# Attention outputs per head in two column halves of the TensorE array, written in one burst per unit

## The reference, cut to what matters

```python
def _attn_ref(q, k, v):                       # B, H, S, D = 4, 8, 576, 64
    q_d, k_d, v_d = (means over 4 neighbouring rows of q, k, v)      # 144 rows each
    out_d  = softmax(q_d @ k_d.T / 8) @ v_d                          # coarse, 144 keys
    mask   = np.abs(pos[:, None] - pos[None, :]) < 4
    out_local = softmax(where(mask, q @ k.T / 8, -1e9)) @ v          # a band of 7 keys
    return np.repeat(out_d, 4, axis=2) + out_local

def reference(...):
    x = attention output as (B*S, H*D) = (2304, 512)
    h = x @ w_in;  g = max(h, 0) + alpha * min(h, 0);  y = g @ w_out         # 512 -> 2048 -> 512
    h = y @ w2_in; u = h if h > 0 else exp(h) - 1;     return u @ w2_out     # 512 -> 2048 -> 512
```

## Time and profile before

| what | before |
|---|---|
| median of three runs | 945.79 us (945.70 to 945.86) |
| the profiled execution | 946.88 us, span 945.1 us |
| PE, PEld busy | 934.2, 882.3 us |
| DVE, ACT, POOL busy | 566.5, 328.8, 285.3 us |
| granted PE clock | 1.0 in every slice |

### The profile page before, as it was taken

How to read it: one execution, slowest core, us unless ns; L and a number is a source line. 1 busy time by engine, 2 the same in 40 slices (tenths; PEclk the granted TensorE clock), 3 DMA queues, 4 the chain that set the end, 5 groups by cost and what they waited for, 6 DMA issues and landing times.

```text
span 945.1 us, 15299 instructions
## 1 busy us (share of the span) xinstructions
PE 934.2 (99%) x5615; PEld 882.3 (93%) x5620; DVE 566.5 (60%) x1100; ACT 328.8 (35%) x756; POOL 285.3 (30%) x395
## 2 busy tenths in 40 slices
PE   8999999999999999999999999999999999999998
PEld 6999999999999999999999998888888888898887
DVE  5875666665565555445446566565856566756563
ACT  5853334333342313133232123232533233523233
POOL 3898952222112225455457552110001100000000
PEclk9999999999999999999999999999999999999999
DMA  7755522211211103536335234434454444454411
GB/s 168 166 146 142 144 72 53 52 41 40 50 41 39 28 16 112 156 107 195 101 134 201 60 119 112 122 112 119 116 180 122 112 122 113 153 149 112 122 45 68
DMA packets 119834, 100.70 MB, mean 107 GB/s; under 512 B 66000, under 2 KB 82384, under 8 KB 119760
## 3 DMA queue, kind: packets, MB, share of 16 engines
q1 hardware_dynamic: 118576, 99.42, 37.6%
q10 hardware_dynamic: 1184, 0.30, 0.2%
HBM read 80.29 MB, written 19.40 MB: 105 GB/s over the span
## 4 chain that ended last, share of the span: by engine, by line
PE 90%; POOL 5%; issue 2%; DVE 2%; ACT 1%; DMA 1%; SPq 0%; DVEq 0%; POOLq 0%; ACTq 0%
PE ps L236 27%; PE ps L237 26%; PE ps L238 26%; PE ps L469 3%; PE ps L436 2%; PE ps L461 1%; POOL w_out_lo L718 1%; POOL w_in_lo L718 1%; PE ps L418 1%; PE ps L426 1%; POOL p_l L692 1%; POOL vd L684 1%; PE ps L443 1%; PE ps L451 1%; POOL p_c L689 1%
## 5 line engine op out<-in xcount | busy, mean ns | idle before, releaser
L238 PE MATMUL ps<-common,w_hi 128*128 128x384 f32 x768 | 258.2, 336 | 0.0
L237 PE MATMUL ps<-common,w_hi 128*128 128x384 f32 x768 | 257.9, 336 | 0.0
L237 PEld LDWEIGHTS ps<-common,w_hi 128*128 128x128 f32 x768 | 144.7, 188 | 0.0
L238 PEld LDWEIGHTS ps<-common,w_hi 128*128 128x128 f32 x768 | 144.3, 188 | 0.0
L311 ACT ACTIVATE common<-act_g 128x384 fp32r<-128x384 f32 x96 | 50.4, 525 | 245.8 <-PE ps L238 125.5
L236 PE MATMUL ps<-common,w_out_lo 128*128 128x384 f32 x384 | 132.7, 346 | 0.4 <-DVE common L315 0.4
L236 PE MATMUL ps<-common,w_in_lo 128*128 128x384 f32 x384 | 132.6, 345 | 0.0
L869 ACT ACTIVATE act_g<-act_g 128x384 f32<-128x384 f32 x96 | 50.5, 526 | 196.0 <-DVE act_g L865 196.0
L236 PE MATMUL ps<-w_hi,common 128*128 128x512 f32 x288 | 113.8, 395 | 1.7 <-ACT xT L324 1.0
L238 PE MATMUL ps<-w_hi,common 128*128 128x512 f32 x288 | 113.5, 394 | 0.0
L237 PE MATMUL ps<-w_out_lo,common 128*128 128x512 f32 x288 | 113.5, 394 | 0.0
(11 more groups left out here) (103 smaller groups left out, 1615.2 us busy)
## 6 DMA issues: line engine op xcount, KB each, us to landing
ring<-w_in_parts SPq DMA_DIRECT2D x168, 256.0 KB, 2.7
w_in_parts<-parts SPq DMA_DIRECT2D x8, 1280.0 KB, 5.7
qk_nat<-in_q SPq DMA_DIRECT2D x32, 144.0 KB, 2.8
v_nat<-in_v SPq DMA_DIRECT2D x16, 288.0 KB
out<-xT SPq DMA_DIRECT2D x18, 256.0 KB, 2.2
qk_nat<-in_k SPq DMA_DIRECT2D x30, 144.0 KB, 3.3
v_blk<-in_v SPq DMA_DIRECT2D x64, 67.5 KB
xT<-in_moe_w_in SPq DMA_DIRECT2D x16, 256.0 KB, 3.0
```

The costliest lines, as they stand in the source:

```text
L237: pe.matmul(psum, l_hi, r_lo, start=False, stop=False)
L238: return pe.matmul(psum, l_hi, r_hi, start=False, stop=stop)
```

## The change

For each head the outputs are computed in one half of the array's columns: head 0 writes partitions 0 to 63 of the result and head 1 partitions 64 to 127, for the coarse and for the local part.

- `v_win` replaces `v_blk`: v as it is, 64 columns per head as stationary operand, windows padded from 54 to 64 partitions (`KP`). The zero blocks move to the probabilities: `pT_l` gets a side dimension, and the moving operand has 2 x 48 columns, of which each window sees its own. `vd` holds one copy.
- A matmul of the local outputs has 64 stationary and 96 moving columns (128 and 48 before), one of the coarse outputs 64 and 144 (128 and 144 before). Their numbers stay: 12 and 4 a unit. In the built program they stand on tiles of 128 x 64 of the array, at column 0 for head 0 and at column 64 for head 1, taking turns; all other matmuls stay on 128 x 128.
- `OUTPUTS` becomes two jobs, `O` 0 (coarse and the first block of 2 x 96 columns) and `O` 1 (the other two blocks), and `bursts` never splits them. The step has 13 jobs instead of 14, still seven bursts.
- DVE: `copy_coarse` is one operation of 128 x 144, `write_x` one of 128 x 192 for `O` 0 and two for `O` 1. In the mixed part `sum_local` and `reciprocals` of unit u + 1 stand ahead of `copy_coarse` at `O` 0.
- ACT: `copy_pT_local` has two operations of 64 partitions instead of one of 108. The high parts of the weights leave ACT.
- POOL: `sum_v` has three operations instead of four. `hi_of_weights` is on POOL for all chunks, in two operations of 512 columns (one of 1024 on POOL before).

```diff
-            v_blk = sb("v_blk", [2 * KW, NWH, HEADS, 2, D])
-            vd = sb("vd", [SC, HEADS, 2, 2, D])
+            v_win = sb("v_win", [2 * KP, NWH, HEADS, D])
+            vd = sb("vd", [SC, HEADS, 2, D])
...
-            pT_c, pT_l = sb("pT_c", [SC, 2, NW, HEADS, DQ]), sb("pT_l", [2 * KW, NWH, HEADS, QW])
+            pT_c, pT_l = sb("pT_c", [SC, 2, NW, HEADS, DQ]), sb("pT_l", [2 * KP, NWH, 2, HEADS, QW])
...
-                for h in range(HEADS):
-                    for x in range(2):
-                        last = pe.matmul(ps[:, bank, h * SD:(h + 1) * SD], vd[:, h, x, :, :].rearrange("p o d -> p (o d)"),
-                                         pT_c[:, x, :, h, :], start=x == 0, stop=x == 1)
-                last.then_inc(oc_done, 1)
-
-            def output_local(pe, u, h, bank):
-                pe.wait_ge(v_win_loaded, V_LOADS * (u + 1))
-                pe.wait_ge(ptl_copied, 2 * u + 2)
-                for i in range(NWH):
-                    last = pe.matmul(ps[:, bank, QW * i:QW * (i + 1)],
-                                     v_blk[:, i, h, :, :].rearrange("p s d -> p (s d)"), pT_l[:, i, h, :],
-                                     start=True, stop=True)
-                last.then_inc(ol_done, 1)
+                for x in range(2):
+                    for h in range(HEADS):
+                        pe.matmul(ps[D * h:D * (h + 1), bank, 0:SD], vd[:, h, x, :], pT_c[:, x, :, h, :], start=x == 0,
+                                  stop=x == 1)
+
+            def output_blocks(pe, u, n, bank):
...
+                for j in range(NBH):
+                    if block_at(j)[0] == n:
+                        for i in (2 * j, 2 * j + 1):
+                            for h in range(HEADS):
...
+                                last = pe.matmul(to, v_win[:, i, h, :], pT_l[:, i, :, h, :], start=True, stop=True)
+                last.then_inc(o_done, 1)
...
-                elif kind == "OC":
-                    copy_coarse(dve, u)
-                    if BATCH_UNITS <= u and u + 1 < UNITS:
-                        if u + 2 == UNITS:
-                            sum_local(dve, u + 1, 0)
-                        sum_local(dve, u + 1, 1)
-                        reciprocals(dve, u + 1)
-                elif kind == "OL":
+                elif kind == "O":
+                    if i == 0:
+                        if BATCH_UNITS <= u and u + 1 < UNITS:
+                            if u + 2 == UNITS:
+                                sum_local(dve, u + 1, 0)
+                            sum_local(dve, u + 1, 1)
+                            reciprocals(dve, u + 1)
+                        copy_coarse(dve, u)
                     write_x(dve, u, i)
...
-            def hi_of_weights(act, c):
-                act.wait_ge(w_loaded[c % WS], 32 * (c // WS + 1))
-                act.activation(w_hi[:, :, c, :], w_stage[:, c % WS, :, :], ACT.Copy).then_inc(w_hi_done, 1)
+            def hi_of_weights(gp, c):
+                gp.wait_ge(w_loaded[c % WS], 32 * (c // WS + 1))
+                for which in range(2):
+                    last = gp.tensor_scalar(w_hi[:, which, c, :], w_stage[:, c % WS, which, :], 1.0, 0.0, ALU.mult, ALU.add)
+                last.then_inc(w_hi_done, 1)
```

More of the change, by code:

```diff
@@ L171, in bursts @@
         grouped = [jobs[sum(sizes[:n]):sum(sizes[:n + 1])] for n in range(len(sizes))]
[L172 removed]
+        burst = []
+        for job in jobs[sum(sizes):]:
+            if len(burst) == 2 or burst and job[1:3] == OUTPUTS[0]:
+                grouped.append(burst)
+                burst = []
+            burst.append(job)
+        return grouped + [burst]
     with ExitStack() as ctx:
```

131 lines of the change are left out of this document (67 added, 64 removed).

## The result

| | before | after |
|---|---|---|
| median | 945.83 us (945.70 to 945.87, 4 runs) | 932.58 us (931.34 to 933.37, 4 runs) |
| profiled execution, span | 946.88, 945.1 us | 933.14, 931.3 us |

The ratio is 0.9859, with a 95% interval of 0.9842 to 0.9876. The forecast of 931.0 us is 1.6 us off and the range holds the time, but not every step behind it was right: two large ones were wrong in opposite directions. The kernel before ran 38 times beside this kernel and those of the experiments; seven of these executions took 948.9 to 950.2 us at a mean granted clock of 0.996 to 0.998, the others 945.4 to 946.5, and none of the seven was profiled.

The account below looks back on a forecast made before the run. PE, busy 934.2 of 945.1 us, was taken as the bound except in units 0 to 3 and at unit 5's wait. 946.88 - 16.8 (outputs) + 0.8 (POOL) + 1.2 (clock) = 932.1; median 1.1 lower, 931.0 us; range 923 to 942.5.

Parts of the forecast that it names:

- I take 53 and 60 ns: PE's local and coarse output records: halves stream side by side, weight loads follow each other; 1.76 us a unit, chance 0.40.
- the first rival: PE's outputs: loads and streams both side by side, 40 and 60 ns a record; 927.4 us, 922.6 without drains and clock; chance 0.18.
- Changing to halves and back, 0.33 us: PE around a unit's outputs: pipeline runs empty at each change, 0.16 us in and out, bounds 0 and 0.33.
- Units 0 to 3 save nothing: Attention alone: the loop setting the pace leaves the outputs out, so shorter outputs save nothing there.
- the attention alone still at 9.6 us: Units 0 to 3 running alone: each step was to stay at 9.6 us; movement would show the prediction wrong.
- POOL +0.8: POOL from 53.37 to 79.29, ahead of unit 5's transposes: changed operations add 0.8 us, bounds 0 and +2.
- PE's pause of 4.1 us, price 1.2: PE ahead of unit 5's transposes: idle about 4.1 us, lower clock then costs 1.2 us, bounds 0 and 2.4.
- DVE and ACT at nothing, under PE: Their changed work runs beside PE and costs nothing; without that cover ACT's copies would cost 0.6 us a unit.
- Normalising late: Rival: denominators one burst later delay transposes in later units; 935.5 us if missed by 0.5 us on nine units; chance 0.08.
- Taking turns: Rival on PE's outputs: halves alternate, 80 and 120 ns a record, 2.88 us a unit; 942.1 us, chance 0.17.
- loads not run ahead: Slower rival on PE's outputs: a record costs load and stream, 133 and 173 ns, halves taking turns; 961 us, chance 0.07.
- The sum: Whole kernel: 946.88 less 16.8 for outputs, plus 0.8 for POOL and 1.2 for the clock, 932.1 us profiled.

Follow-up runs that it names:

- e1: Changed kernel with all output matmuls of head 0 ahead of those of head 1 in each job, instead of taking turns; 934.42 us in one run.
- e7: e3 with a unit's two output jobs in bursts of their own in the mixed tiles, products between them; 931.80 us, ratio 0.9853.
- e2: Kernel before the change without its idle-filling bf16 matmuls behind the outputs of units 0 to 2; 949.78 us in one run.
- e3: Changed kernel with seven instead of one useless bf16 matmul behind the second output job of units 0 to 2; 929.60 us, ratio 0.9817.
- e10: e9 with the last denominators and reciprocals on DVE one burst ahead of the outputs in the mixed part; 921.06 us, ratio 0.9724.
- e4: Changed kernel with late weight chunks handed out 3, 5, 4, 0 to units 4 to 7 instead of 4 each for units 4 to 6; 930.33 us.
- e5: e3 with 28 useless matmuls in PE's pause ahead of unit 5's first transposes; 927.97 us, ratio 0.9816.
- e8: e3 with late weight chunks handed out 3, 4, 5, 0 to units 4 to 7; 926.03 us, ratio 0.9796.
- e9: e8 with high parts as before the change: chunks 0 to 3 on ACT, others on POOL in one operation of 1024 columns; 923.35 us, ratio 0.9759.
- e6: e3 with high parts as before the change: chunks 0 to 3 on ACT, others on POOL in one operation of 1024 columns; 928.90 us, ratio 0.9817.
- e11: The changed kernel run once more, unaltered; 934.40 us in one run.

## Why the prediction came out right, point by point

- **"I take 53 and 60 ns"** was wrong for the local outputs. They take 41 ns a record, the first rival's number; the coarse ones 61. The step that failed is that the loads of both halves follow one another because every load before is a single stream of records. The single stream of loads was what the whole array showed, and in halves it is not there. e1 gives both numbers: 82 ns for a half alone, 41 with two.
- **Changing to halves and back, 0.33 us**: the mechanism was right, the size 0.26 by the records, and e7 has it as time. A unit saves 1.90 instead of 1.53 us, eleven of them 20.9 instead of 16.8. The Trainium skill's rule in "TensorEngine Tiling (Array Packing)", Tiling Modes, that a change of mode drains the engine agrees with these records in that each change costs time. Each way costs less than the 0.16 us taken for a pipeline that runs empty (0.15 in, 0.11 out): the next record starts 0.07 us before the modelled end of the last one on either way.
- **"Units 0 to 3 save nothing" and "the attention alone still at 9.6 us"**: the first half was true, the second false, and it was the most expensive of the misses that made the kernel slower, 3.2 us. I had asked what the loop waits for and not what the shorter outputs leave behind: a pause of 1.40 us a step, whose price is the clock of the scores, 2.9 us. e2 and e3 show it from both sides. The other 0.3 us are POOL's added high parts, which the prediction let vanish in POOL's pause of 1.29 us a step.
- **POOL +0.8**: it was +0.42. The wait for chunk 7's load, 1.16 us in the earlier trace rows, did not stay: in after nothing is waited for at 78.57. In return the high part there took 1.53 us (1.20 elsewhere) and the low parts 0.2 us more in sum; why is not shown.
- **PE's pause of 4.1 us, price 1.2**: it was 5.64 us and 2.03. The direction was right and the price inside its bounds (0 to 2.4); the middle was mis-sized. The 1.5 us more of pause are 0.4 for the larger saving of unit 4's outputs, 0.7 because PE's first product stands 1.8 us earlier against unit 4's normalising (1.1 was taken), and 0.7 because PE's waits on DVE ahead of unit 5 shrank from 0.42 and 0.59 us to one of 0.32, less 0.4 for POOL.
- **DVE and ACT at nothing, under PE**: this failed, for 1.46 us in three waits at changes of tile. DVE's work did fall, but its order cost 0.75 us, which e10 takes away. I had looked at the sum of its work and at the denominators' effect on POOL, and not at who else stands behind them on DVE. The other 0.71 us are ACT's copies, which the prediction named and took to be covered: they take 0.97 us more a unit (1.68 instead of 0.71), not 0.6, and at one place the cover of 0.28 us was too short.
- **Rivals.** Normalising late did not come: unit 6's starts at 108.25 and PE needs it at 110.42 in the chain; unit 7's at 131.97, with the transposes at 134.66. It had room of 1.3 and 1.8 us behind POOL's 0.91, near the 1 us estimated. Taking turns (942.1) and loads not run ahead (961) are excluded by the 41 ns. The Trainium skill's rule in "TensorE: Matmul & The Clock Gate", Part 3, The mechanism, that loads overlap only where row groups differ, is not borne out: both halves use all rows, and their records cost what streaming costs. The same section of the Trainium skill also lets a load into a background weight buffer run ahead, and with that these records do not conflict.
- **The sum.** Against 932.1 for the profiled run it is off by -4.1 (outputs), +3.2 (attention alone), +0.8 (clock at unit 5), +1.5 (waits on DVE, half of it through ACT) and -0.4 (POOL): +1.0, to 933.1. The forecast was right because its misses offset each other, not because each term was.

## What to carry to other kernels

When a change makes the dominant engine's work shorter at a place where it is not the bound, ask what the pause that it leaves does: here it lowered the clock of work that was the bound, and six more matmuls of no use a step gave 3 us back. When operations are gathered into one burst, look on the engines that serve it at what now stands right behind them, above all where one tile follows another; an engine that is busy for 36% of the span, as ACT, can still be late at one place. And two short waits cost less here than one long one, since the clock stayed up: levelling the side engine's load (chunks 3, 4, 5 in place of 4, 4, 4) gave 3.6 us, shortening it alone gave 0.7, and shortening it once it was levelled gave 2.7.

## What the runs showed of the hardware

- Two column halves of the array run plain f32 matmuls side by side, loads included: pairs start 7 ns apart, and a pair costs what one record costs (82 ns for 96 moving columns, as in one half alone in e1; 122 for 144, as in the whole array). Order in the program matters little: with all of one half first the cost rose by 0.34 us in 32 records, since by their start times PE ran records of the other half ahead (e1).
- Going into halves and back cost 0.26 us each time, besides the 0.09 that any f32 burst has behind it.
- After single pauses of 0.87 to 1.80 us in front of PE's transposes the granted clock stayed at its upper level (e4, e5, e8, e9, e10). With pauses of 2.51 us (e4, unit 6), 3.61 (e6), 4.76 (e7) and 5.3 to 5.6 us (e1, after, e3, e11) it fell to the lower. The cost was not in order of the pause but of the work that fell into the stretch at the lower level: 6.3 us of it cost 2.92 us (e6, pause 3.61), 3.4 us of it 1.56 (e3, pause 5.62).
- With a pause of 1.4 us in every 9.7 us step, the clock fell in some steps and executions and not in others; with the pause filled it did not in the traces of the seven kernels that had it filled (e3, e5 to e10).
- A copy on ACT of 288 columns took 0.41 us for 64 partitions and for 108, so cutting one copy into two by height doubled its time.
